# A fused convolution and two feed-forward layers: order of work on VectorE, ScalarE and TensorE

## What is computed

```
w   = softmax(weight)                    # 8 heads x 7 taps
x1  = causal convolution of x over 7 tokens, a set of taps for each head
h   = x1 @ w_in1                         # 192 -> 2048
g   = (a0 + a1 h + a2 h^2 + a3 h^3) / (1 + |b0| |h| + |b1| h^2 + 1e-6)
x2  = g @ w_out1                         # 2048 -> 192
r   = max(x2 @ w_in2, 0)                 # 192 -> 2048
out = (s r^2 + b) @ w_out2               # 2048 -> 192
```

## Time and profile before

| | |
|---|---|
| runs shown | 1279.95, 1281.68, 1279.95 us (median 1279.95) |
| the profiled execution's own time | 1280.64 us |
| its span, first to last instruction | 1278.8 us |
| mean granted TensorE clock | 0.996 of full speed |
| TensorE matmul busy | 1258.7 us (98%) |
| VectorE busy | 1131.6 us (88%) |
| ScalarE busy | 1105.5 us (86%) |
| GpSimd busy | 330.5 us (26%) |

### The profile page before, as it was taken

One profiled execution on the slowest core, in us unless ns is written; L12 is line 12 of the kernel. 1 busy time (PEld: TensorE's weight loads), 2 busy tenths in 40 slices (PEclk: granted clock), 3 DMA queues, 4 the chain that ended last, 5 costly groups with the idle time before them and its releaser, 6 DMA issues.

```text
span 1278.8 us, 16225 instructions
## 1 busy us (share of the span) xinstructions
PE 1258.7 (98%) x5986; PEld 1070.4 (84%) x5986; DVE 1131.6 (88%) x1047; ACT 1105.5 (86%) x1074; POOL 330.5 (26%) x153
## 2 busy tenths in 40 slices
PE   7999999999999999999999999999999999999999
PEld 4758888888888888888888888888888888888888
DVE  7997899998999989998999989999899998889750
ACT  6898888898898988988898888989889888888853
POOL 3342222322322222222223222222222222232220
PEclk9998999999999999999999999999999999999999
DMA  7100000010000100000000100001000000000000
GB/s 232 49 17 9 1 14 1 1 38 1 12 0 12 25 0 12 0 25 13 0 12 0 37 0 12 0 0 37 0 12 0 12 0 1 13 1 14 1 13 13
DMA packets 14604, 20.39 MB, mean 16 GB/s; under 512 B 1776, under 2 KB 9968, under 8 KB 14320
## 3 DMA queue, kind: packets, MB, share of 16 engines
q1 hardware_dynamic: 14432, 20.01, 5.4%
q10 hardware_dynamic: 144, 0.01, 0.0%
HBM read 13.72 MB, written 6.29 MB: 16 GB/s over the span
## 4 chain that ended last, share of the span: by engine, by line
PE 75%; DVE 13%; issue 6%; POOL 2%; ACT 2%; DMA 1%; SPq 0%; DVEq 0%; ACTq 0%; POOLq 0%
PE o L441 21%; PE o L413 4%; PE h L392 4%; PE h L433 4%; PE h L434 4%; PE h L424 4%; PE h L423 4%; PE h L396 4%; PE o_tail L414 4%; PE h L393 4%; PE h L395 4%; PE h L394 4%; PE h L428 4%; PE o_tail L407 3%; PE o L405 3%
## 5 line engine op out<-in xcount | busy, mean ns | idle before, releaser
L381 POOL TENSOR_TENSOR gl<-work,gh 128x1024 fp32r<-128x1024 f32 x128 | 308.4, 2410 | 848.0 <-ACT gh L642 784.6
L441 PE MATMUL o<-v,work 128*128 128x192 f32 x2048 | 353.3, 326 | 0.0
L441 PEld LDWEIGHTS o<-v,work 128*128 128x128 f32 x2048 | 339.2, 190 | 9.9
L835 DVE SCALAR_TENSOR_TENSOR work<-work,coef,h 128x1024 f32<-128x1024 f32 x128 | 163.7, 1279 | 76.1 <-ACT work L637 73.4
L665 ACT ACTIVATE work<-work 128x1024 f32<-128x1024 f32 x128 | 136.0, 1063 | 58.0 <-DVE work L835 56.5
L636 ACT ACTIVATE work<-h,coef 128x1024 f32<-128x1024 f32 x128 | 154.0, 1203 | 30.8 <-PE h L396 28.2
L873 DVE SCALAR_TENSOR_TENSOR work<-work,coef 128x1024 f32<-128x1024 f32 x128 | 164.5, 1285 | 4.5
L841 DVE SCALAR_TENSOR_TENSOR work<-work,coef,h 128x1024 f32<-128x1024 f32 x128 | 164.0, 1281 | 4.5
L669 ACT ACTIVATE work<-h 128x1024 f32<-128x1024 f32 x128 | 131.2, 1025 | 40.4 <-PE h L434 37.7
L867 DVE SCALAR_TENSOR_TENSOR work<-work,coef 128x1024 f32<-128x1024 f32 x128 | 163.8, 1280 | 0.5
L869 DVE SCALAR_TENSOR_TENSOR work<-work 128x1024 f32<-128x1024 f32 x128 | 159.0, 1242 | 4.4
(11 more groups left out here) (87 smaller groups left out, 2012.1 us busy)
## 6 DMA issues: line engine op xcount, KB each, us to landing
out_dram<-y_out SPq DMA_DIRECT2D x32, 192.0 KB, 2.0
xt<-in_x_main_dram SPq DMA_DIRECT2D x7, 518.0 KB, 5.3
xt_tail<-in_x_tail_dram SPq DMA_DIRECT2D x8, 259.0 KB, 5.5
work<-in_moe_w_out_dram SPq DMA_DIRECT2D x1, 1536.0 KB, 9.3
v<-in_moe_w_out_dram SPq DMA_DIRECT2D x1, 1536.0 KB, 8.3
raw_w_tail_late<-in_moe_w_in_dram SPq DMA_DIRECT2D x4, 256.0 KB, 8.6
work<-in_moe_w_in_dram SPq DMA_DIRECT2D x2, 512.0 KB, 5.6
xt<-in_x_main_dram SPq DMA_DIRECT2D x2, 259.0 KB, 5.3
```

The source lines that it names most:

```text
L381: nc.gpsimd.tensor_tensor(gl[:, j % 2, :], r_buf[j % 2], gh[:, j % 2, :].bitcast(F32), ALU.subtract).then_inc(gl_ready, 1)
L441: return pe.matmul(o2[:, c // 2, c % 2, 0:D], g, v2[:, f, :], start=(f == 0 and c % 2 == 0), stop=(f == FT - 1), skip_group_check=True)
L835: nc.vector.scalar_tensor_tensor(q_buf[buf], w_of_n, b0_abs, h_flat, ALU.add, ALU.mult).then_inc(z_done, 1)
```

## The change

Four edits. On TensorE, at step j = 3 (`X2_STEP + 1`), the two matmuls of the high part of layer 2's first product, half 0, are issued ahead of layer 1's product, behind a wait for `u_ready`; the later call does the rest. On ScalarE the logarithm stands ahead of the relu and square, and in the steady state it writes w_abs instead of r_buf; the wait for `gl_ready` moves to the exponential, and the first steps of the next unit wait for the exponential (`r0_ready`), as they overwrite w_abs. On VectorE the three instructions of g stand ahead of the splits and the taps.

```diff
-            def first_product_of_layer_2(k, x2p, t2):
+            def high_part_of_layer_2(k, x2p, half):
+                c = slice((2 * k + half) * P, (2 * k + half + 1) * P)
+                pe.matmul(h2[:, half, :], w2_hi[:, c], x2_hi[x2p][:, :], start=True, stop=False)
+                pe.matmul(h2[:, half, :], w2_lo[:, c], x2_hi[x2p][:, :], start=False, stop=False)
+
+            def first_product_of_layer_2(k, x2p, t2, halves):
...
-                for half in range(2):
-                    pe.matmul(h2[:, half, :], w2_hi[:, c[half]], x2_hi[x2p][:, :], start=True, stop=False)
-                    pe.matmul(h2[:, half, :], w2_lo[:, c[half]], x2_hi[x2p][:, :], start=False, stop=False)
+                for half in halves:
+                    high_part_of_layer_2(k, x2p, half)
...
+                    part_ahead = j == X2_STEP + 1 and unit(m) and unit(n)
+                    if part_ahead:
+                        pe.wait_ge(u_ready, counted(m))
+                        high_part_of_layer_2(k2, x2p, 0)
                     if unit(n) and not (isinstance(n, int) and n <= SKEW):
                         product_of_layer_1(n, j, t, parity)
...
-                        first_product_of_layer_2(k2, x2p, t2)
+                        first_product_of_layer_2(k2, x2p, t2, (1,) if part_ahead else (0, 1))
```

```diff
                         act.wait_ge(t3_done, counted(n))
+                        act.wait_ge(r0_ready, counted(n))
                         first_steps(n, h1_flat, t_buf, w_abs)
...
+                    ln_of_n = r_buf[buf] if ahead(n + 1) else w_abs
+                    if unit(n):
+                        act.wait_ge(q_ready, counted(n + 1))
+                        if ahead(n + 1):
+                            act.wait_ge(gl_ready, counted(n - 1))
+                        nc.scalar.activation(ln_of_n, q_buf[buf], ACT.Ln, bias=one_eps).then_inc(ln_done, 1)
                     if unit(m):
                         act.wait_ge(h2_ready, counted(m + 1))
...
-                    if unit(n):
-                        act.wait_ge(q_ready, counted(n + 1))
-                        act.wait_ge(gl_ready, counted(n - 1))
-                        nc.scalar.activation(r_buf[buf], q_buf[buf], ACT.Ln, bias=one_eps).then_inc(ln_done, 1)
...
-                        nc.scalar.activation(r_buf[buf], r_buf[buf], ACT.Exp, scale=-1.0).then_inc(r0_ready, 1)
+                        act.wait_ge(gl_ready, counted(n - 1))
+                        nc.scalar.activation(r_buf[buf], ln_of_n, ACT.Exp, scale=-1.0).then_inc(r0_ready, 1)
```

More of the change, by code:

```diff
@@ L537, in phase @@
                     early = isinstance(n, int) and n < SKEW
+                    x2p = (parity + (j - SKEW) // UNITS) % 2
+                    part_ahead = j == X2_STEP + 1 and unit(m) and unit(n)
+                    if part_ahead:
+                        pe.wait_ge(u_ready, counted(m))
+                        high_part_of_layer_2(k2, x2p, 0)
                     if unit(n) and not (isinstance(n, int) and n <= SKEW):
@@ L566, in phase @@
                             pe.wait_ge(t3_done, n)
-                        x2p = (parity + (j - SKEW) // UNITS) % 2
-                        first_product_of_layer_2(k2, x2p, t2)
+                        first_product_of_layer_2(k2, x2p, t2, (1,) if part_ahead else (0, 1))
                     ends_layer_1 = not tile(t) and j == OUT1_LAG - 1
@@ L665, in phase @@
                         nc.scalar.activation(q_buf[buf], q_buf[buf], ACT.Abs).then_inc(q_ready, 1)
+                    if ahead(n + 1) and n > 0:
+                        act.wait_ge(t3_done, 1 if n == 1 else n + 1)
+                        first_steps(n + 1, h2_flat if in_h2(n + 1) else h1_flat, t_buf, w_abs)
+                    ln_of_n = r_buf[buf] if ahead(n + 1) else w_abs
[4 more added lines that the diff above has]
+                        nc.scalar.activation(ln_of_n, q_buf[buf], ACT.Ln, bias=one_eps).then_inc(ln_done, 1)
                     if unit(m):
@@ L672, in phase @@
                         nc.scalar.activation(g2[buf], u_relu, ACT.Square).then_inc(g2_ready, 1)
-                    if ahead(n + 1) and n > 0:
-                        act.wait_ge(t3_done, 1 if n == 1 else n + 1)
-                        first_steps(n + 1, h2_flat if in_h2(n + 1) else h1_flat, t_buf, w_abs)
-                    if unit(n):
-                        act.wait_ge(q_ready, counted(n + 1))
-                        act.wait_ge(gl_ready, counted(n - 1))
-                        nc.scalar.activation(r_buf[buf], q_buf[buf], ACT.Ln, bias=one_eps).then_inc(ln_done, 1)
                     if cast_early(n - 1):
@@ L852, in phase @@
                                 ALU.mult, ALU.add).then_inc(y_ready_out, 1)
+                    q, r, num = q_buf[1 - buf], r_buf[1 - buf], num_buf[1 - buf]
+                    if unit(n - 1):
+                        dve.wait_ge(r0_ready, counted(n))
+                        nc.vector.scalar_tensor_tensor(q, q, one_eps, r, ALU.add, ALU.mult).then_inc(e_done, 1)
+                        dve.wait_ge(e_done, counted(n))
+                        nc.vector.scalar_tensor_tensor(r, q, 2.0, r, ALU.subtract, ALU.mult,
+                                                       reverse0=True).then_inc(r1_done, 1)
+                        dve.wait_ge(r1_done, counted(n))
+                        dve.wait_ge(t3_done, counted(n))
+                        nc.vector.scalar_tensor_tensor(r, num, a0, r, ALU.add, ALU.mult).then_inc(g_ready, 1)
                     if tile(t) and pair_exists(i + 1) and (parity, j) == at(i, SPLIT_A, SPLIT_A_FIRST):
@@ L862, in phase @@
                             tail_tap(k, i + 1, tail_steps(i) + k)
[L864 to L873, removed]
                     if first(t) and j == 4:
```

## The result

The changed kernel takes 1294.38 us (median of 5 runs, 1294.01 to 1295.82), the kernel before 1281.12 us beside it. The ratio of after to before is 1.0109 with a 95% interval of 1.0097 to 1.012: slower by 1.1%. 1295 was forecast. The profiled execution took 1294.01 us, its span is 1292.2 us, 13.4 more than before.

The account below looks back on a forecast made before the run. TensorE's own work, 9.42 us a steady unit, was taken as the bound. Terms +12.9 - 1.6 + 3.6 = +14.9 us on 1280.64 gave 1295.5 profiled, stated as 1295; range 1287 to 1301 (forecast's own 1289 to 1300).

Parts of the forecast that it names:

- TensorE is the bound, and single units pay: Steady units take 9.42 us of TensorE's own work; an edit can give back only the excess round sums and splits.
- Part 1, the relu behind the logarithm: At 14 sums the moved matmuls wait for the later relu: 0.72 us each, 0.92 with line 413's lateness, +12.9 us.
- The second term, line 413 of the next unit: Behind a sum, two matmuls fewer before line 413 make gl late: 0.2 us a sum, bounds 0 and 0.35.
- the first term: At each sum, moved matmuls wait for the relu and line 392 starts later: net loss 0.72 us.
- rival (b): Faster: at the 14 sums the moved matmuls find the relu done; -7.2 us, 1273, or 1277 with the ramp's cost; chance 0.07.
- The added wait of the first steps: ScalarE's lines 636 and 637 wait for the exponential: cost 0, about 0.1 us where ScalarE is full.
- Part 2, g ahead: At 7 splits of parity 1 g comes earlier, -0.23 us each, -1.6 us; nothing gained at parity 0.
- The tap units: In units with taps, g held gh by hundredths only, so g ahead was priced at 0.
- The ramp: At unit 5's split GpSimd's line 338 and gl block VectorE: 3.6 us lost, bounds -0.3 and 3.7, or 5.
- Rival (a): The relu is late, but the split's instructions slip between GpSimd's, so the ramp costs nothing: 1291.4 us; chance 0.18.
- rival (c): The longer stalls at the 14 sums lower TensorE's clock, 45 us or more: over 1325 us; chance 0.05.

Follow-up runs that it names:

- e1: The changed kernel with the logarithm moved back behind the relu and square on ScalarE: 1281.82 us, ratio to the kernel before 1.0012.
- e2: The changed kernel without the two matmuls ahead, all else kept: 1281.83 us, ratio to the kernel before 1.0012.
- e3: The changed kernel with the ramp's split (unit 5) put back ahead of g on VectorE: 1292.04 us, ratio to the kernel before 1.0089.
- e6: The changed kernel with one more wait on GpSimd, at unit 6, for the ramp's split: 1291.63 us, ratio to the kernel before 1.0092.
- e12: The kernel before with ScalarE's new order alone (logarithm in w_abs ahead of the relu, added wait for the exponential): 1282.38 us, ratio 1.0017.
- e4: The kernel before with VectorE's new order alone (g ahead of splits and taps): 1280.8 us, ratio 1.0006.
- e7: The kernel before with g ahead of splits and taps, except at the ramp's split: 1277.47 us, ratio 0.9981.
- e10: The kernel before with g first (not at the ramp's split), gl in halves, four matmuls ahead at parity 0, two at parity 1: 1274.11 us, ratio 0.9954.

## Why the prediction was right

**TensorE is the bound, and single units pay.** Right. Nearly all that changed in the stretch is at the 14 sums and 7 splits; the other units together are some 0.6 us shorter.

**Part 1, the relu behind the logarithm.** Right in place, number and size. 14 sums of tiles 2 to 15 stall 0.72 to 0.81 us at the moved matmuls, and the relu is what they wait for; the working had 562.28 less 557.77 = 4.51 from z to the first matmul ahead, measured 4.53. e1 and e2 show that it takes both edits. The sum of tile 1, priced at nothing, stalled 0.40 as well. There the relu ended 4.61 behind z in the changed kernel, in e3 and in e6 alike, but TensorE waited 0.40, 0.95 and 0.17: the longest in e3, where the granted clock stayed at 1.00 and TensorE came there soonest behind z.

**The second term, line 413 of the next unit.** 0.2 was taken for the lateness of gl. Measured, line 413 stands 5.89 behind the block at 570.64, 0.11 late, and with the refill and the slower matmuls behind it costs 0.25; the first term, foreseen at 0.72, cost 0.73. Together 0.92 a sum was forecast and 0.98 to 1.00 measured. What the prediction did not draw out is that this term stands against the moved matmuls whatever the relu does. Its faster rival (b) priced the gain at 0.34 of parity 1's stall and 0.46 of parity 0's with no such term, 1273 or 1277 us. e1 shows that case, the ramp's cost with it: 1281.8 us, no faster than before. The step that failed in (b) is the cover of line 413, priced in the forecast and left out of the rival.

**The added wait of the first steps.** Taken at 0, or 0.1 where ScalarE is full. It is 0.17 long at a sum, and ScalarE's part alone costs 2.6 us of stretch (e12), nearly half of it in units that the working held to be covered. In the changed kernel it is covered at the sums, as h1 comes later still; of the sum, nothing of it shows.

**Part 2, g ahead.** Right: -0.24 at the split of parity 1, nothing at parity 0 (e4, e7). The tap units were priced at 0 and gave some hundredths each, which the sums of parity 1 took back: e4's stretch is 1.75 shorter, and the 7 splits alone give 1.7.

**The ramp.** The mechanism was right, its size a little high: 3.04 us on VectorE (12.80 from z to z against 9.76), 3.6 taken. The first cast of the split started before GpSimd, and the last subtraction after gl, so less than the full length of both was lost. Of it 1.8 us came through up to the first block in that execution: the inputs were 0.5 us sooner (z of unit 5 at 55.27, before at 55.76), and the low granted clock at the first sum took less away (mean 0.50 from 98 to 104 us before, 0.72 after). The spans of e3 and e6 are 1.7 and 2.6 us shorter than the changed kernel's.

The Trainium skill, "SBUF — State Buffer", "Who interferes with whom", lets GpSimd block a fast VectorE copy, or an instruction with two inputs in SBUF, for a whole instruction. The changed kernel and e6 bear that out: the 2.75 us subtraction ended 0.55 behind gl's end (67.32 against 66.77), the 1.40 us cast 0.27 behind the end of line 338 (64.53 against 64.26), each less than the 0.69 and 0.42 that the two take undisturbed, and both are short when GpSimd waits.

**Sum.** +12.9 - 1.6 + 3.6 = 14.9 was forecast; the profiled execution grew by 13.4 (11.6 in the stretch, 1.8 up to the first block). That the forecast time of 1295 came within 0.6 of the measured one has some luck in it: the growth was forecast 1.5 too high, and the kernel before had a median of 1279.95 in the three runs shown but of 1281.12 in all five. Rival (a), a ramp that does not pay, is ruled out by e3 and e6, and rival (c), a lower clock, by the clock row above.

## What to carry to other kernels

Two edits that each cost little or nothing can cost a percent together: where one edit makes an engine wait for a step sooner, look at every other edit that makes this step later. Work moved in front of a stall is taken from in front of the next wait, so ask which wait lost its cover; here the move paid only when the next producer, gl, was cut in two so that its first half was ready 1.1 us sooner. Where an engine sets the pace, mind what else wakes at the same semaphore: an instruction moved ahead freed GpSimd into the middle of VectorE's fast work.

## What the runs showed of the hardware that was not expected

A matmul behind a stall takes about 0.33 us to its successor, and the ten or so behind it are 0.23 to 0.24 apart and not 0.227, also where no wait is shown; this makes part of the excess of e10, and its cause stays open. GpSimd's gl in two halves takes 2.56 us for both against 2.41 in one, and this cost nothing to be seen. At the first sum, behind a pause of TensorE of 2.35 us, the granted clock was 0.50 from 98 to 104 us in the kernel before, and 1.00 from 94 to 106 us in e3, where the pause was 2.35 too: the length of this pause alone doesn't decide it. Executions of one kernel differ as well: of the 67 of the kernel before beside the experiments, 12 have a mean granted clock of 0.996 and spans of 1279.2 to 1280.2 us, 41 have 0.997 and 1277.4 to 1279.2, so a difference of a microsecond between two profiled executions is within that. The stalls of 0.72 to 0.81 at the later sums never lowered it.
